# Identity transposes in the waits of the start, and the last chunk handed from engine to engine in halves

## The reference

```python
w = exp(weight_gen - max(weight_gen)); w = w / (sum(w) + 1e-09)      # over the 7 taps
x_unf = x_pad[:, idx, :].reshape(B, S, K, H, group)                 # batch 2, seq 4096, width 192
x = einsum('bshk,bskhg->bshg', w, x_unf).reshape(8192, 192)
h = maximum(x @ w_in, 0);  x = (h * h) @ w_out                      # width 192 -> 2048 -> 192
h = x @ w_in2;             out = (h * cos(h)) @ w_out2              # 192 -> 2048 -> 192
```

## Time and profile before

| | us |
|---|---|
| median of 3 runs | 1194.85 |
| the runs | 1194.55, 1194.85, 1198.56 |
| the profiled execution's own time | 1197.12 |
| its span in the profile | 1195.3 |
| TensorE busy in it | 1174.2 (98%) |
| VectorE, ScalarE, GpSimd busy | 964.0, 815.5, 365.8 |
| mean granted clock of TensorE | 0.996 |

### The profile page before, as it was taken

The page is one execution under the profiler, slowest core; times in us unless marked ns, Lnnn a source line. Parts: engine busy times, 40 slices in busy tenths (PEclk is TensorE's granted clock), DMA queues, the critical chain, the costliest instruction groups (busy, mean ns, idle before and its releaser), DMA issues.

```text
span 1195.3 us, 25441 instructions
## 1 busy us (share of the span) xinstructions
PE 1174.2 (98%) x9768; PEld 1107.3 (93%) x9768; DVE 964.0 (81%) x1503; ACT 815.5 (68%) x1488; POOL 365.8 (31%) x265
## 2 busy tenths in 40 slices
PE   6999999999999999999999999999999999999998
PEld 4978999899999999999999999999999999999976
DVE  7867888978878787787878878787787878878787
ACT  3987675766667676676766666666666767666675
POOL 3894706061250704206060240705216070000000
PEclk8999999999999999999999999999999999999999
DMA  7422111011111111111001111101111000100000
GB/s 191 116 67 48 35 27 34 10 19 35 28 34 18 28 23 23 34 27 35 12 17 35 27 34 22 35 13 22 34 28 34 13 16 3 26 1 15 1 15 14
DMA packets 113172, 37.30 MB, mean 31 GB/s; under 512 B 101662, under 2 KB 110878, under 8 KB 113052
## 3 DMA queue, kind: packets, MB, share of 16 engines
q1 hardware_dynamic: 111100, 34.87, 13.9%
q10 hardware_dynamic: 1952, 0.80, 0.3%
HBM read 23.84 MB, written 6.29 MB: 25 GB/s over the span
## 4 chain that ended last, share of the span: by engine, by line
PE 90%; DVE 5%; ACT 3%; issue 1%; DMA 0%; SPq 0%; ACTq 0%; DVEq 0%
PE y L593 47%; PE h L593 43%; DVE h L1345 1%; DVE h L1367 1%; DVE g_lo L1380 1%; DVE turns L1349 1%; ACT turns L1076 1%; ACT g_hi L1089 1%; ACT relu L1049 0%; ACT arena L1032 0%; DMA xc<-in_x_dram 0%; DVE x L1322 0%; ACT gen L1038 0%; DVE stat L1205 0%; DVE stat L1196 0%
## 5 line engine op out<-in xcount | busy, mean ns | idle before, releaser
L593 PE MATMUL y<-g_hi,wo 64*128 64x512 f32 x3048 | 699.4, 395 | 0.6 <-DVE y_part L1389 0.4
L593 PE MATMUL y<-g_lo,wo 64*128 64x512 f32 x2032 | 526.2, 393 | 0.0
L593 PEld LDWEIGHTS y<-g_hi,wo 64*128 64x128 f32 x3048 | 423.4, 184 | 27.2 <-PE y L593 5.1
L514 POOL TENSOR_TENSOR tap<-xc,gen 128x768 f32<-128x768 f32 x98 | 150.9, 1546 | 581.9 <-DVE xd_lo L1357 566.3
L593 PEld LDWEIGHTS y<-g_lo,wo 64*128 64x128 f32 x2032 | 309.0, 184 | 4.8
L1076 ACT ACTIVATE turns<-turns 128x512 f32<-128x512 f32 x238 | 150.4, 632 | 197.1 <-DVE turns L1349 196.2
L593 PE MATMUL h<-xa_hi,wa_hi 64*128 64x512 f32 x1016 | 273.9, 400 | 2.9 <-issue 2.4
L593 PE MATMUL h<-xa_lo,wa_hi 64*128 64x512 f32 x1016 | 269.8, 393 | 0.2 <-DVE g_lo L1239 0.2
L593 PE MATMUL h<-xa_hi,wa_lo 64*128 64x512 f32 x1016 | 268.2, 391 | 0.0
L1367 DVE TENSOR_TENSOR h<-h,turns 128x512 f32<-128x512 f32 x238 | 165.9, 697 | 122.5 <-ACT turns L1076 121.6
L1345 DVE SCALAR_TENSOR_TENSOR h<-h,relu 128x512 f32<-128x512 f32 x249 | 173.4, 697 | 66.2 <-ACT relu L1049 63.6
(11 more groups left out here) (117 smaller groups left out, 1093.8 us busy)
## 6 DMA issues: line engine op xcount, KB each, us to landing
xc<-in_x_dram SPq DMA_DIRECT2D x60, 240.0 KB
out_dram<-arena SPq DMA_DIRECT2D x62, 64.0 KB, 1.9
xt_a<-x_blocks SPq DMA_DIRECT2D x224, 16.0 KB, 1.8
arena<-in_moe_w_out_dram SPq DMA_DIRECT2D x16, 192.0 KB, 3.1
arena<-in_moe_w_in_dram SPq DMA_DIRECT2D x16, 128.0 KB, 2.4
out_dram<-arena SPq DMA_DIRECT2D x62, 32.0 KB, 1.7
xt_d<-x_blocks SPq DMA_DIRECT2D x112, 16.0 KB, 1.8
arena<-in_moe_w_in_dram SPq DMA_DIRECT2D x16, 64.0 KB, 2.9
```

The costliest lines, as they stand in the source:

```text
L514: pool.tensor_tensor(tap[:, k % 2, :].rearrange("p (r g) -> p r g", g=GROUP), rows[k], wk, ALU.mult).then_inc(pool_step, 1)
L593: return pe.matmul(o, w[rows, :], x[rows, :], start=start, stop=stop)
```

## The change

At the start, the turns of the identity go through a function `keep_busy(count)` and write to bank 3 of `h`. There are now 8 behind the first product, 7 behind the second, 8 behind each of the first three sums, 14 (8 and 6) behind the fourth, 2 between the two parts of `turn_x1`, and 3 in slot 0 between the second and the third weight product (L619 and L622). In all 58 stand where 40 stood.

At the end, chunk 255 is cut into two halves of 256 tokens (`parts`), each in a bank of its own, and every step from its up products to its down products works by halves. Its slot on TensorE is a new function, `last_tail_up`.

```diff
+            def keep_busy(count):
+                for _ in range(count):
+                    pe.transpose(h[:, 3, 0:P], ident[:, :], ident[:, :])
...
             pe.matmul(o, wa_lo[l][:, f_cols], xa_hi[l][:, par, :], start=False, stop=False)
             if first:
+                keep_busy(3)
                 pe.wait_ge(x1_split, 1)
...
             pe.wait_ge(ident_ready, 2)
-            pe.wait_ge(first_product, 1)
-            for k in range(TAPS - 2):
-                if k:
-                    pe.wait_ge(first_sum, k)
-                for _ in range(WARM_UP):
-                    pe.transpose(h[:, 0, 0:P], ident[:, :], ident[:, :])
+            for k in range(2):
+                pe.wait_ge(first_product, k + 1)
+                keep_busy(8 - k)
+            for k in range(1, TAPS - 2):
+                pe.wait_ge(first_sum, k)
+                keep_busy(8)
+            keep_busy(6)
             pe.wait_ge(first_sum, TAPS - 1)
             turn_x1(0, 0)
+            keep_busy(2)
             pe.wait_ge(first_sum, TAPS + 1)
             pe.wait_ge(pad_zeroed, 1)
             turn_x1(0, 1)
...
+        def parts(m):
+            count = 2 if m == STEPS - 1 else 1
+            return [(k, slice(k * TOK // count, (k + 1) * TOK // count)) for k in range(count)]
...
             def last_down(k, y, l, f, hi, lo):
...
+                for part, cols in parts(k):
+                    part_a, part_d = y[:, 0, cols], y[:, 1, cols]
+                    pe.wait_ge(g2_hi_ready, k + 1 + part)
+                    pe.matmul(part_a, w[:, f, 0:DA], hi[:, cols], start=False, stop=False)
+                    pe.matmul(part_a, w[:, f, 2 * P:2 * DM], hi[:, cols], start=False, stop=False)
+                    pe.matmul(part_d, w[:, f, DA:2 * P], hi[:, cols], start=False, stop=False)
...
+                (_, cols), (_, cols2) = parts(k)
                 pe.wait_ge(g2_ready, k + 1)
+                pe.matmul(y[:, 0, cols], w[:, f, 0:DA], lo[:, cols], start=False, stop=False)
+                pe.matmul(y[:, 1, cols], w[:, f, DA:2 * P], lo[:, cols], start=False, stop=False)
+                pe.wait_ge(g2_ready, k + 2)
+                pe.matmul(y[:, 0, cols2], w[:, f, 0:DA], lo[:, cols2], start=False, stop=True).then_inc(down2_done, 1)
+                pe.matmul(y[:, 1, cols2], w[:, f, DA:2 * P], lo[:, cols2], start=False, stop=True).then_inc(y2_d_done, 1)
...
+            def last_tail_up(m, k):
...
+                up_a(o, 1, f, of, BOTTOM, 2, cols)
+                up_d(o, 1, f, of, 0, cols)
+                pe.wait_ge(g2_ready, k + 1)
+                pe.wait_ge(tail_a_done, turn - 1)
+                down_a(down, TOP, 0)
+                up_d(o, 1, f, of, 2, cols).then_inc(h2_left, 1)
+                pe.wait_ge(g2_ready, m - 2)
+                up_a(o2, 1, f, of, BOTTOM, 0, cols2, start=True)
...
+                up_a(o, 1, f, of, TOP, 2, cols)
+                up_d_top(o, f, cols, stop=True).then_inc(up2_done, 1)
...
+                up_a(o2, 1, f, of, TOP, 2, cols2)
+                up_d_top(o2, f, cols2, stop=True).then_inc(up2_done, 1)
+                down_d(down, BOTTOM, 1).then_inc(down2_done, 1)
...
             def tail_chunk(m):
...
+                    for part, cols in parts(m):
+                        act.wait_ge(up2_done, m + 1 + part)
+                        act.activation(turns[:, c, cols], h[:, tail_bank(m + part), cols], ACT.Copy,
+                                       bias=0.25).then_inc(turns_ready, 1)
...
+                    for part, cols in parts(m - 1):
+                        act.wait_ge(g2_made, m + part)
+                        act.activation(g2_hi[:, 1 - c, cols], h[:, tail_bank(m - 1 + part), cols],
+                                       ACT.Copy).then_inc(g2_hi_ready, 1)
```

More of the change, by code:

```diff
@@ L245, in conv_ffn_ffn_kernel @@
         block = ctx.enter_context(nc.Block())
-        WARM_UP = 8
         LATE = 4
@@ L730, in end_of_tail_up @@
                 up_d_top(h[:, tail_bank(m), :], f, stop=True).then_inc(up2_done, 1)
+            def last_tail_up(m, k):
+                f, of = m % SLOTS, m // SLOTS % 2
+                (o, cols), (o2, cols2) = [(h[:, tail_bank(m + part), :], at) for part, at in parts(m)]
+                down = (y1, 1, k % SLOTS, g2_hi[:, k % 2, :], g2_lo[:, k % 2, :])
+                turn = k - (TAIL - LAG - TAIL_D2) + 1
+                up_a(o, 1, f, of, BOTTOM, 0, cols, start=True)
+                up_a(o, 1, f, of, BOTTOM, 1, cols)
+                end_of_tail_up(m - 1)
+                up_a(o, 1, f, of, BOTTOM, 2, cols)
+                up_d(o, 1, f, of, 0, cols)
+                pe.wait_ge(g2_ready, k + 1)
+                pe.wait_ge(tail_a_done, turn - 1)
[3 more added lines that the diff above has]
+                up_a(o2, 1, f, of, BOTTOM, 0, cols2, start=True)
+                down_a(down, TOP, 1)
+                up_a(o2, 1, f, of, BOTTOM, 1, cols2)
+                up_a(o2, 1, f, of, BOTTOM, 2, cols2)
+                down_a(down, TOP, 2).then_inc(tail_a_left, 1)
+                up_d(o2, 1, f, of, 0, cols2)
+                up_d(o2, 1, f, of, 2, cols2).then_inc(h2_left, 1)
+                pe.wait_ge(down2_done, k)
+                down_d(down, TOP, 0)
+                pe.wait_ge(h2_left, m)
+                up_a(o, 1, f, of, TOP, 0, cols)
+                up_a(o, 1, f, of, TOP, 1, cols)
+                pe.wait_ge(tail_a_left, turn)
+                down_a(down, BOTTOM, 0)
+                up_a(o, 1, f, of, TOP, 2, cols)
+                up_d_top(o, f, cols, stop=True).then_inc(up2_done, 1)
+                down_a(down, BOTTOM, 1)
+                down_d(down, TOP, 1).then_inc(tail_d_left, 1)
+                down_a(down, BOTTOM, 2).then_inc(tail_a_done, 1)
+                pe.wait_ge(h2_left, m + 1)
+                up_a(o2, 1, f, of, TOP, 0, cols2)
+                up_a(o2, 1, f, of, TOP, 1, cols2)
+                pe.wait_ge(tail_d_left, turn)
+                down_d(down, BOTTOM, 0)
+                up_a(o2, 1, f, of, TOP, 2, cols2)
+                up_d_top(o2, f, cols2, stop=True).then_inc(up2_done, 1)
+                down_d(down, BOTTOM, 1).then_inc(down2_done, 1)
             def tail_slot(n):
@@ L746, in tail_slot @@
                         pe.wait_ge(x2_split, TILES)
+                    if m == STEPS - 1:
+                        last_tail_up(m, k)
+                        return
                     up_a(o, 1, f, of, BOTTOM, 0, start=True)
-                if STEPS - SLOTS < m <= STEPS:
+                if STEPS - SLOTS < m < STEPS:
                     end_of_tail_up(m - 1)
@@ L1231, in tail_chunk @@
                 c = m % 2
-                o = h[:, tail_bank(m), :]
                 if m < STEPS:
-                    dve.wait_ge(turns_ready, m + 1)
-                    dve.scalar_tensor_tensor(wave[:, c, :], o, 0.25, turns[:, c, :], ALU.add,
-                                             ALU.subtract).then_inc(fraction_ready, 1)
+                    for part, cols in parts(m):
+                        dve.wait_ge(turns_ready, m + 1 + part)
+                        dve.scalar_tensor_tensor(wave[:, c, cols], h[:, tail_bank(m + part), cols], 0.25,
+                                                 turns[:, c, cols], ALU.add, ALU.subtract).then_inc(fraction_ready, 1)
                 if m > TAIL - LAG:
-                    dve.wait_ge(g2_hi_ready, m)
-                    dve.tensor_tensor(g2_lo[:, 1 - c, :], h[:, tail_bank(m - 1), :], g2_hi[:, 1 - c, :],
-                                      ALU.subtract).then_inc(g2_ready, 1)
+                    for part, cols in parts(m - 1):
+                        dve.wait_ge(g2_hi_ready, m + part)
+                        dve.tensor_tensor(g2_lo[:, 1 - c, cols], h[:, tail_bank(m - 1 + part), cols],
+                                          g2_hi[:, 1 - c, cols], ALU.subtract).then_inc(g2_ready, 1)
                 if m < STEPS:
-                    dve.wait_ge(cos_ready, m + 1)
-                    dve.tensor_tensor(o, o, wave[:, c, :], ALU.mult).then_inc(g2_made, 1)
+                    for part, cols in parts(m):
+                        o = h[:, tail_bank(m + part), cols]
+                        dve.wait_ge(cos_ready, m + 1 + part)
+                        dve.tensor_tensor(o, o, wave[:, c, cols], ALU.mult).then_inc(g2_made, 1)
                 if m == STEPS - SLOTS + 2:
```

43 lines of the change are left out of this document (16 added, 27 removed).

## The result

| | before | after |
|---|---|---|
| median of 22 runs, us | 1195.76 | 1193.84 |
| lowest and highest | 1194.21, 1199.80 | 1193.45, 1195.50 |
| ratio, with its 95% interval | | 0.9981 (0.9973 to 0.9989) |
| the profiled execution's own time | 1197.12 | 1193.82 |
| its span | 1195.3 | 1192.0 |

The account below looks back on a forecast made before the run. The prediction took TensorE, 90% of the chain of waits, to bound the kernel, leaving gains only at the two ends. From 1197.12 us it took 2.7 (start) and 0.7 (end), giving 1193.7, range 1192.4 to 1197.2.

Parts of the forecast that it names:

- The first term: Start, slots 1 to 3: added turns keep TensorE at 2.4 GHz; 2.42 us from slots 1 and 2, 0.33 from slot 3.
- What the forecast said of the runs: Fast runs of the kernel before hardly lose the clock; the change removes slow ones, and the median moves by 1.1 us.
- All of it reaches the end: Behind slot 3: the whole 2.7 us gets through, 2.0 by room at slot 6, 0.7 by VectorE moving up.
- The rival of the head: Fourth rival, behind slot 3: the head gives 0.7 us back to VectorE, total 1194.4 us; chance 0.05.
- the lower bound that I gave for this term: Start: 2.0 us of the 2.7 gained if VectorE's work in the head did not move up.
- The turns cost nothing: Start: the 18 added turns delay nothing at 0.11 us each, hidden behind VectorE's sums and waits; cost 0.
- the second rival: Start: turns at 0.20 us delay turn_x1 by up to 0.65 us, low clock persists; 1197.3 us, chance 0.07.
- The rule against it: Start: by the Trainium skill, transposes do not count as clock activity like matmuls, making the first term 0 instead of 2.7.
- The end: Last chunk in halves: last down product near 1189.45 instead of 1190.35, 0.9 us ahead, taken as 0.7; VectorE sets the chain.
- The allowance that I made for hand-overs: End: gain taken as 0.7 us instead of 0.9, for estimated hand-overs and 0.11 us on the first product after a pause.
- The stretch that I had named as its sign: End: last up product to last down product should take 4.2 us instead of 4.9, with VectorE working without a pause.
- The third rival: End: weight loads do not overlap products, the 7 last take 0.2 us each, 0.6 us is lost; 1194.3 us, chance 0.10.

Follow-up runs that it names:

- The shift of the convolution product: Changed kernel with one VectorE convolution product moved from behind slot 2 to behind slot 3; median 1193.43 us, changed kernel beside it 1193.99.
- the end alone: Changed kernel with its turns put back to the 40 of before, only the last chunk in halves; median 1194.23 us.
- only the late turns: Changed kernel without the 7 turns behind the second product, the 6, 2 and 3 late ones kept; median 1194.07 us.
- the start alone: Kernel before with only the turns of the identity changed, its end as before; median 1194.56 us, kernel before beside it 1197.08.
- the 2 and the 3: Halves at the end and the 40 turns of before, plus keep_busy(2) and keep_busy(3) without the 6; median 1193.93 us.

## Why the prediction was right

*The clock.* The first term, 2.7 us for slots 1 to 3, was right in kind and 0.3 us too small: slots 1 and 2 gave 2.70 us where 2.42 were forecast. They take 1.79 and 1.69 us, not 1.88. The step from the third product to the first on 64 rows is 0.33 us in them, where the sum took the 0.43 of slot 0, and slot 3's first product, on 64 rows like the one ahead of it, follows after 0.23 instead of 0.32. The rest of slot 3 gave 0.3 on top, as forecast: ScalarE's operation L1117 stands 3.2 us earlier than before at 25.6 us and 3.5 at 30.8. What the forecast said of the runs is borne out as well. In the three sets of 35 runs of the kernel before that were taken beside the experiments, those near 1194.5 have a mean clock of 0.998 or 0.999 and the others 0.993 to 0.996, and the median of the nearest upper group lies 2.3 to 2.6 us above that of the low one. Against the low group the changed kernel wins only the end's share.

*All of it reaches the end.* This step failed in size. The rival of the head came true beside the forecast: 0.5 to 0.8 us went back, 0.4 of them where slot 6 waits for VectorE's low part of slot 3 (the same operation of ScalarE stands 3.1 us earlier than before at 36.5 us), 0.3 more near slot 9 (2.85 from 41.7 us on), and 0.2 only near 1144 us. I had counted on VectorE to move up by the missing 0.7 us; its low part of slot 3 moved from 33.88 to 32.73, 1.15 us, of which 0.49 is the earlier input. The shift of the convolution product, which took this wait away, shows it: there ScalarE's operations keep their 3.1 us from 29 us until near 1148. The sum of 3.4 us stayed right only by luck, because the input came 0.49 us earlier in the second profile, which no step had foreseen. The runs show it too: the profiled execution before, 1197.12, lies 0.4 us above the median of its own group (1196.73), and from this group to the low one of the changed kernel it is 2.9 us, not 3.4. Set against the lower bound that I gave for this term, 2.0, the measured 2.2 (2.67 less 0.49) is nearer than the 2.7 taken.

*The turns cost nothing.* Right: 0.11 us each at the high clock, and `turn_x1` waits for VectorE. At the low clock they cost 1.0 us at the first transpose, where the second rival had 0.65. Its price of 14 times 0.20 left out that the first weight load of the tile's transposes comes 0.33 us behind the last one of the turns. At slot 1 it was 0.9, which equals the rival's sum of 0.9 only because the clock had risen on the way. In neither profile of the changed kernel was the clock low at 16 us. With the early 7 turns missing it can be: in the profile of the end alone, 32 turns from 11.26 us on took 6.72 us. But the eleven runs of "only the late turns", which leave the 7 out as well, show no cost.

*The rule against it.* The Trainium skill (TensorE: Matmul & The Clock Gate, Part 4, PE-mode transpose) has it that transposes do not count as activity in the way that matmuls do. The runs say the opposite here: with 16 turns and the tile's transposes alone the clock is up at slot 0's first product (20.89 us, 0.34 to the next), without the turns it is not (0.57 to the next). And with 5 turns in the last gaps no run of 12 fell into the groups above 1196, where without them 4 of 12 did, and 7 of 12 with 6 turns ahead of the tile's first transpose.

*The end.* 0.7 us forecast; 0.74 measured from chunk 254's product and 0.69 from chunk 255's first up product, and 0.5 to 0.7 between low groups of runs taken side by side. The working had the wrong engine last: I let the second high half start at 1188.43 behind VectorE, 3.24 us behind chunk 254's product, and it started at 3.44, because TensorE still had the first half's three products. The allowance that I made for hand-overs covered the 0.2 us. The stretch that I had named as its sign, from the end of the last up product to that of the last down product, did not come out: 4.2 us were forecast and 4.43 measured (1182.56 to 1186.99), against 4.93 before. So 0.5 us of the gain lie behind the last up product and 0.2 ahead of it: the 18 up products of 256 columns took 2.50 us, the nine of 512 took 2.69. Their weight loads, which I had put at nothing, added nothing. The third rival, that weight loads keep the halves from gaining, falls with products 0.12 us apart.

*The median.* 1193.84 against 1193.7, and it moved by less than half a per cent, as forecast. It moved by 1.9 us and not by 1.1, because the median before is no firm mark: it was 1194.85 in the first 3 runs, 1195.76 when they had become 22, and 1197.08, 1194.77 and 1196.91 in three further sets of 35, according to how many of them fell.

Open is what decides in which executions of the kernel before the clock falls, why the early turns alone make it fall in all, and in which executions it falls at 60 us.

## What to carry to other kernels

When runs of one kernel lie in groups, look at the clock in the first microseconds of dense work before comparing medians; the gain of a change may be that it takes the upper group away. Fill the last gaps ahead of the dense work, not only an early one: with the last gaps filled no run was above 1196 in four of these kernels (the start alone, the changed kernel, only the late turns, the 2 and the 3), and with the early gap alone filled all twelve were. When a stage gets faster, ask at once which engine's operation stands ahead of the one that is waited for, and try the single move: it gave 0.5 us here, about as much as cutting the last chunk.

## What was not expected of the hardware

Turns of the identity raise the clock and hold it: with 16 of them and 16 small transposes from 16.24 us on it was up at 20.89 us, in eight of ten runs by their times. The granted clock reads 1.00 ahead of its first recorded change, also where the products stand 0.42 us apart, at 1.2 GHz. And behind a pause of 1.4 us, 60 us into the program, with TensorE busy before and after it, the clock fell in one profile, and that execution was 1.4 us longer than the median.
